# Sliding-window attention run inside the chunks of the first of two MLPs, with x kept on chip

## The reference

```python
# q, k, v: (4, 8, 576, 64) fp32; window 64
scores = q @ k.T / sqrt(64);  keep 0 <= i - j < 64, else -1e9
attn = exp(scores - max) / (sum + 1e-9);  o = attn @ v
x = o, heads beside each other: (2304, 512)
xn = x / sqrt(mean(x * x) + 1e-6) * rms_g
g = xn @ w_gate;  x2 = (g * sigmoid(g) * (xn @ w_val)) @ w_out     # 512 -> 1536 -> 512
h = x2 @ w_in;    out = (h * sigmoid(1.702 * h)) @ w_out2          # 512 -> 2048 -> 512
```

## Time and profile before

| | |
|---|---|
| runs | 1022.56, 1022.61, 1025.49 us |
| profiled execution, first to last instruction | 1025.4 us |
| PE busy | 982.7 us (96%) |
| DVE, ACT, POOL busy | 416.3, 349.5, 136.5 us |
| mean granted TensorE clock | 0.992 of 2.4 GHz |
| DMA | 58.29 MB, queue busy 20.2% of 16 engines' span |
| chain that ended last | PE 84%, DVE 7%, issue 4%, ACT 2%, DMA 1% |

### The profile page before, as it was taken

How to read it: one execution, slowest core, us unless ns; L and a number is a source line. 1 busy time by engine, 2 the same in 40 slices (tenths; PEclk the granted TensorE clock), 3 DMA queues, 4 the chain that set the end, 5 groups by cost and what they waited for, 6 DMA issues and landing times.

```text
span 1025.4 us, 15826 instructions
## 1 busy us (share of the span) xinstructions
PE 982.7 (96%) x5584; PEld 930.4 (91%) x5584; DVE 416.3 (41%) x797; ACT 349.5 (34%) x950; POOL 136.5 (13%) x90
## 2 busy tenths in 40 slices
PE   6887888999999999999999998999999999999998
PEld 5777778999999999999999997998999899999997
DVE  5989986653323332332333342222232322322322
ACT  5877876322112122122122342232232222322322
POOL 3343364620000000000001652000000000000000
PEclk9999999999999999999999998999999999999999
DMA  8656762512002002002003332010010010100000
GB/s 169 142 146 163 166 178 83 157 31 70 0 0 69 0 0 69 0 0 69 0 0 123 123 124 82 1 54 8 0 61 0 0 61 0 61 0 0 31 0 31
DMA packets 98603, 58.29 MB, mean 57 GB/s; under 512 B 59664, under 2 KB 90128, under 8 KB 98576
## 3 DMA queue, kind: packets, MB, share of 16 engines
q1 hardware_dynamic: 98576, 57.95, 20.2%
HBM read 42.60 MB, written 15.34 MB: 57 GB/s over the span
## 4 chain that ended last, share of the span: by engine, by line
PE 84%; DVE 7%; issue 4%; ACT 2%; DMA 1%; SPq 1%; DVEq 0%; POOL 0%; ACTq 0%
PE ps L589 21%; PE ps L591 21%; PE ps L590 21%; PE ps L674 6%; PE ps L676 6%; PE ps L675 6%; DVE nmax L882 1%; DVE probT L906 1%; DVE rrec L891 1%; DVE vwin L918 1%; ACT prob L718 1%; DVE prob L897 1%; DVE xT L244 1%; DVE rrec L894 1%; DMA wstage<-in_moe_w_out 1%
## 5 line engine op out<-in xcount | busy, mean ns | idle before, releaser
L589 PE MATMUL ps<-x_hi,w_main 128*128 128x384 f32 x672 | 226.2, 337 | 0.0
L591 PE MATMUL ps<-x_lo,w_main 128*128 128x384 f32 x672 | 225.6, 336 | 0.0
L590 PE MATMUL ps<-x_hi,w_main 128*128 128x384 f32 x672 | 225.5, 336 | 0.0
L1004 DVE TENSOR_TENSOR hid<-ps,sig 128x384 f32<-128x384 f32 x96 | 53.5, 558 | 295.1 <-ACT sig L835 295.0
L835 ACT ACTIVATE sig<-ps 128x384 f32<-128x384 f32 x96 | 47.2, 492 | 281.2 <-PE ps L591 281.2
L771 ACT ACTIVATE sig<-ps 128x384 f32<-128x384 f32 x72 | 35.4, 492 | 301.0 <-PE ps L591 301.0
L589 PEld LDWEIGHTS ps<-x_hi,w_main 128*128 128x128 f32 x672 | 126.5, 188 | 3.1
L590 PEld LDWEIGHTS ps<-x_hi,w_main 128*128 128x128 f32 x672 | 126.4, 188 | 2.8
L591 PEld LDWEIGHTS ps<-x_lo,w_main 128*128 128x128 f32 x672 | 126.4, 188 | 0.0
L970 DVE TENSOR_TENSOR sig<-ps,sig 128x384 f32<-128x384 f32 x72 | 40.1, 557 | 210.9 <-ACT sig L771 210.9
L589 PE MATMUL ps<-x_hi,w_tail 128*128 128x384 f32 x288 | 97.0, 337 | 0.0
(11 more groups left out here) (87 smaller groups left out, 1612.9 us busy)
## 6 DMA issues: line engine op xcount, KB each, us to landing
wstage<-in_moe_w_out SPq DMA_DIRECT2D x28, 256.0 KB, 3.5
xstage<-xs_scratch SPq DMA_DIRECT2D x6, 960.0 KB, 5.9
xs_scratch<-xT SPq DMA_DIRECT2D x16, 288.0 KB, 2.2
xs_scratch<-ostage SPq DMA_DIRECT2D x6, 768.0 KB, 3.9
xstage<-xs_scratch SPq DMA_DIRECT2D x6, 768.0 KB, 4.5
out_dram<-ostage SPq DMA_DIRECT2D x18, 256.0 KB, 2.0
qraw<-in_q SPq DMA_DIRECT2D x30, 144.0 KB, 3.0
kraw<-in_k SPq DMA_DIRECT2D x30, 144.0 KB, 3.2
```

What stands on the lines that cost most here:

```text
L589: pe.matmul(out_, w[:, 0, cols], xh, start=first, stop=False)
L590: pe.matmul(out_, w[:, 1, cols], xh, start=False, stop=False)
L591: return pe.matmul(out_, w[:, 0, cols], xl, start=False, stop=last)
L1004: nc.vector.tensor_tensor(hid[:, f % 2, :], ps[:, H_BANK + f % 2, 0:T], sig[:, f % 2, :], ALU.mult).then_inc(hidB_made, 1)
```

## The change

**Layout.** q, k, v and the weights are laid out on the host: q block-diagonal for its pair of heads (`q_bd`), k transposed (`k_t`), v as windows of 128 keys for each block (`v_win`), weights by chunk (`w_a`, `w_b`). The transposes of q and k on PE, their evictions on ACT and the copies of v on DVE are gone. The scale of 1/8 goes into the exponential and, by one more small DVE operation, into the row maximum.

**Attention.** A step has 256 queries (4 blocks of 64) of a pair of heads, across batch borders; there are 36. Only the first 4 steps (256 tokens) run before the MLPs. There POOL normalises. The other 32 run inside the chunks of the first four tiles of A, 8 a tile, in chunks 1 to 8: scores between gate and val, transposes before the projection, product with v after it. ACT loads the table of exponentials and that of the sigmoid once in each such chunk. In chunk 10 the sum of squares, the inverse norm and the scaling of the next tile follow.

**x.** Attention's output stays in `xT` in SBUF, is scaled in place, and isn't stored or loaded again. The x2 of A still goes through DRAM.

**Tiles.** A has tiles of 256, 512, 512, 512, 512 tokens, B 512, 512, 512, 512, 256. `sig` and `hid` are single, gate and val have one bank each, and `h_hi` and `h_lo` have three slots.

**Weights.** All twelve slots are split by POOL (cast, `weights_hi_A`, `weights_hi_B`) and DVE (subtraction, `weights_lo_A`, `weights_lo_B`), one of the three parts at a time, none on ACT.

All Python loops are unrolled, the evictions of x2 and of the output are shared by ACT and DVE, and `dynamic_dma_scratch_size` is 1024. The core of the diff, by parts:

```diff
-    GB = 3
...
-    T = 384
-    TILES = TOK // T
...
+GB = 4
...
+    TILES_A = ((0, 256), (256, 512), (768, 512), (1280, 512), (1792, 512))
+    TILES_B = ((0, 512), (512, 512), (1024, 512), (1536, 512), (2048, 256))
+    NA, NB = len(TILES_A), len(TILES_B)
+    TMAX = 512
+    EARLY = 4
...
+    SUMSQ_AT = 10
+    def steps_of(t):
+        return (0, EARLY) if t == 0 else (EARLY + 8 * (t - 1), EARLY + 8 * t)
...
+        w_all = sb("w_all", [P, CA * SLOT], F32R)
+        wstage = sb("wstage", [P, 2 * 3 * DM], F32)
+        x_hi = sb("x_hi", [P, DC, TMAX], F32R)
+        x_lo = sb("x_lo", [P, DC, TMAX], F32R)
...
+        xT = sb("xT", [P, DC, TMAX], F32)
+        h_hi = sb("h_hi", [P, RING, TMAX], F32R)
+        h_lo = sb("h_lo", [P, RING, TMAX], F32R)
+        sig = sb("sig", [P, TMAX], F32)
+        hid = sb("hid", [P, TMAX], F32)
...
+        def x2stage(t):
+            home = wstage if t < NA - 1 else late
+            return home[:, 0:DC * TMAX].rearrange("p (c t) -> p c t", c=DC)
...
+        def o_half(h, s):
             rows = slice(h * BLK, (h + 1) * BLK)
+            group, c = divmod(s, PAIRS)
+            t = 0 if group == 0 else (group + 1) // 2
+            at_ = group * GT - TILES_A[t][0]
+            src = ps[rows, o_bank(s), :].rearrange("p (n k) -> p n k", n=GB)[:, :, h * BLK:(h + 1) * BLK]
+            return t, c, at_, xT[rows, c, at_:at_ + GT].rearrange("p (n r) -> p n r", n=GB), src
+        def evacuate_o(eng, copy, h, s):
+            t, c, at_, dst, src = o_half(h, s)
+            eng.wait_ge(pv_done, s + 1)
+            wait(eng, x_hi_ready, DC * t)
+            wait(eng, x_lo_ready, DC * t)
...
+            def load_wA(c, m):
+                if c >= 2:
+                    sp.wait_ge(w_split, splitsA(c - 2, m))
+                sp.dma_start(raw(c % 2, m), w_a[c, :, m * DM:(m + 1) * DM]).then_inc(w_loaded[c % 2][m], 16)
...
+            for t in range(NA - 1):
+                first, last = steps_of(t + 1)
+                for c in range(CA):
+                    if t == 0 and c + 3 < CA:
+                        for m in range(3):
+                            load_wA(c + 3, m)
+                    s = first + c - FIRST_STEP
+                    if first <= s < last and s + 2 < STEPS:
+                        load_qk(s + 2)
+                    s -= 1
+                    if first <= s < last and s + 2 < STEPS:
+                        load_v(s + 2)
                 store_x2(t)
...
+            def normalise(s):
+                pool.wait_ge(rec_order, 2 * s + 2)
+                by = rrec[:, s % 2, :].rearrange("p (n o) -> p n o", o=1).to_broadcast([P, GB, P])
+                nc.gpsimd.tensor_tensor(prob[:, s % 2, :, :], prob[:, s % 2, :, :], by,
+                                        ALU.mult).then_inc(probs_normed, 1)
...
+            def weights_hi_A(c):
+                for m in range(3):
+                    pool.wait_ge(w_loaded[c % 2][m], 16 * (c // 2 + 1))
+                    nc.gpsimd.tensor_copy(slotA(c)[:, m, 0, :], raw(c % 2, m)).then_inc(w_hi_made, 1)
+            def weights_hi_B(f):
+                pool.wait_ge(projA_done, (NA - 1) * CA + last_slot_under(f) + 1)
+                for m in range(2):
+                    pool.wait_ge(w_loaded[f % 2][m], loadsB(f, m))
+                    nc.gpsimd.tensor_copy(chunkB(f)[:, m, 0, :], raw(f % 2, m)).then_inc(w_hi_made, 1)
...
+            normalise(0)
+            weights_hi_A(0)
+            for s in range(1, EARLY):
+                normalise(s)
+                squares(s - 1)
+            squares(EARLY - 1)
+            weights_hi_A(1)
+            weights_hi_A(2)
+            for t in range(NA - 1):
+                first, last = steps_of(t + 1)
+                for c in range(CA):
+                    s = first + c - FIRST_STEP - 2
+                    if first <= s < last:
+                        squares(s)
+                    if t == 0 and c + 3 < CA:
+                        weights_hi_A(c + 3)
...
+            scores(0)
+            for s in range(EARLY):
+                if s + 1 < EARLY:
+                    scores(s + 1)
+                transpose_probs(s)
+                probs_by_v(s)
+            sum_squares(0)
+            for t in range(NA):
+                first, last = steps_of(t + 1) if t + 1 < NA else (0, 0)
+                for c in range(CA + LAG):
                     if c < CA:
+                        gate(t, c)
+                        s = first + c - FIRST_STEP
+                        if first <= s < last:
+                            scores(s)
+                        val(t, c)
+                    s = first + c - FIRST_STEP - 1
+                    if first <= s < last:
+                        transpose_probs(s)
+                    if c == SUMSQ_AT and last:
+                        sum_squares(t + 1)
+                    if c >= LAG:
...
+                for c in range(CA):
+                    s = first + c - FIRST_STEP
+                    now = first <= s < last
+                    sigmoid_A(t, c)
+                    if now:
+                        nc.scalar.preload_act_table_set(EXP_SET)
+                        exponentials(s)
+                    hid_hi_A(t, c)
+                    if c == SUMSQ_AT and last:
+                        nc.scalar.preload_act_table_set(EXP_SET)
+                        inverse_rms(t + 1)
+                    if now or (c == SUMSQ_AT and last):
...
+            row_max(0)
+            for s in range(EARLY):
+                if s + 1 < EARLY:
+                    row_max(s + 1)
+                reciprocal_of_sum(s)
+                if s >= 1:
+                    evacuate_o(dve, nc.vector.tensor_copy, 0, s - 1)
+                evacuate_probT(s)
+            evacuate_o(dve, nc.vector.tensor_copy, 0, EARLY - 1)
+            weights_lo_A(0)
+            scale_x(0)
             dve.wait_ge(g_loaded, 16)
...
+            for t in range(NA):
+                first, last = steps_of(t + 1) if t + 1 < NA else (0, 0)
+                for c in range(CA):
+                    s = first + c - FIRST_STEP
+                    silu_A(t, c)
+                    if first <= s < last:
+                        row_max(s)
+                    hidden_A(t, c)
+                    if first <= s - 1 < last:
+                        evacuate_probT(s - 1)
+                    if first <= s < last:
+                        normalise(s)
+                    hid_lo_A(t, c)
+                    if first <= s - 1 < last:
+                        evacuate_o(dve, nc.vector.tensor_copy, 0, s - 1)
+                    if t == 0 and c + 2 < CA:
+                        weights_lo_A(c + 2)
+                    if c == SUMSQ_AT and last:
                         scale_x(t + 1)
+                    if t == NA - 1:
+                        for f in range(CB):
+                            if last_slot_under(f) == c - LAG - 1:
+                                weights_lo_B(f)
                 dve.wait_ge(val_done, CA * (t + 1))
...
```

More of the change, by code:

```diff
@@ L230, in evacuate_o, with splitsA @@
[L230 to L245 removed]
+        def splitsA(c, m):
+            return 3 * c + m + 1
@@ new lines, in _ @@
+            load_qk(0)
+            load_wA(0, 0)
+            load_v(0)
+            load_qk(1)
+            load_wA(0, 1)
+            load_v(1)
+            sp.dma_start(gcol[:, :], rms_g).then_inc(g_loaded, 16)
+            for s in range(2, EARLY):
+                load_qk(s)
+                load_v(s)
+                load_wA(0, 2) if s == 2 else load_wA(1, 0)
+            load_wA(1, 1)
+            load_wA(1, 2)
+            load_qk(EARLY)
+            load_v(EARLY)
+            load_qk(EARLY + 1)
@@ L423, in _ @@
[L423 to L428 removed]
+                then(nc.gpsimd.affine_select(out=mask[rows, 3, :], in_=mask[rows, 3, :],
+                                             compare_op=ALU.is_ge, fill=NEG, base=-BLK,
+                                             pattern=[[1, P]], channel_multiplier=0))
@@ L524, in scores, with transpose_probs @@
                                     start=False, stop=True, skip_group_check=True)
                 ins.then_inc(scores_done, 1)
-            def transpose_probs(b, kk):
-                there, j, n = behind(b, kk)
-                if not there:
-                    return
-                pe.wait_ge(probs_normed, n + 1)
-                wait(pe, probT_ready, n)
+            def transpose_probs(s):
+                pe.wait_ge(probs_normed, s + 1)
+                if s < EARLY:
+                    wait(pe, probT_ready, s - 1)
+                else:
+                    for h in range(2):
+                        pe.wait_ge(o_evacuated[h], s)
```

1103 lines of the change are left out of this document (440 added, 663 removed).

## The result

The kernel after takes 981.21 us (median of 4 runs, 979.64 to 981.89) beside 1024.05 for the kernel before on the same chip: ratio 0.9577, 95% interval 0.956 to 0.9594, 4.2% faster. The forecast was 1005 us with a range of 984 to 1026; the direction was right, the size was not, and the time lies 3 us under the range. The profiled execution has a span of 980.1 us.

The account below looks back on a forecast made before the run. PE bounds both MLPs, behind a serial attention of 155 us. Lead 40, MLP matmuls 851.3, steps 83.2, squares 4.0, first tile 20 and 2, tail 3.5, unexplained 4: 1008.0, scaled 1005 us; range 984 to 1026.

Parts of the forecast that it names:

- per column, wider is no cheaper: MLP matmuls: 0.450 and 0.453 ns a column at 384 and 512 columns, so re-tiling gains nothing; 851.3 us in all.
- The 256-column estimate by columns (0.115): MLP matmuls of the 256-token tiles: 0.115 us each, scaled by columns from 384; 624 of them.
- the addition of 1.9 us a chunk for the lock: First tile: POOL's squares and casts meet DVE's subtractions and exclude one another, making a chunk 8.9 us.
- my 20: First tile: PE stalls 17 us over eight chunks, plus 3 while the first splits fill; 20 us.
- the lower bound of 3: First tile's stall if POOL and DVE operations never meet: 3 us.
- about 5.3 each: Lead: the steps after the first, tied through PE's order, add 5.3 us each, from 17 to 33 us.
- The 4 us unexplained: Whole kernel: 1025.4 us profiled before against a calibration of 1021.1; the missing 4 us carried into the forecast.
- rival C: MLP stream: PE waits for normalised probabilities 1.0 us in each of 32 steps, giving 1037 us; chance 0.10.
- rival B: MLP matmuls: 256 columns run at the pace of 384, giving 1024 us; chance 0.08.
- Sums, tail: Sums of squares in the stream: 4.0 us; eviction and store at the end: 3.5 us instead of 3.8.
- the hole's going: Start of the second MLP: ACT's wait for weights goes, and the cold clock with it: 0 us instead of 7.
- rival A: First tile and lead: POOL and DVE interleave without harm, no stall, lead 36 us, scaled 984 us; chance 0.16.

Follow-up runs that it names:

- Fillers: Kernel after with matmuls whose result nobody reads added in the lead to keep PE busy: 974.06 us, ratio 0.9508.
- the new order: Kernel after with the lead's scores two steps ahead, DVE's reciprocal before the next row maximum, an earlier weight load, no filler matmuls: 969.88 us, ratio 0.9458.

## Why the prediction was wrong

**Fixed cost (13.7 of the 27.9 us: 16.8 too much for 512 columns, 3.1 too little for 256).** The step that failed is "per column, wider is no cheaper", worked out from nine matmuls at one place. The same trace held the other reading: in `w_tail` the same form ran at 227 ns, and 384 columns at 173 with 227 gives a constant of 11 to 13 ns. I took a disturbed pace for the pace of the form. A shift of 32 bytes makes the same disturbance in the kernel after; in the kernel before, the distance of `w_tail` brought `w_main` only to 231, so its cause is shown in part. The 256-column estimate by columns (0.115) was off the other way, by 5 ns. The narrow tiles in the second MLP show the constant directly.

The Trainium skill, page "TensorE: Matmul & The Clock Gate", section "Back-to-back issue gap", has the form N/2.4 GHz plus a constant, which I argued away. It gives 2.5 ns, for the isolated gap. The three paces here have this form with 13.3 ns, in a stream with a weight load for every matmul.

**First tile (14.3 us).** The step that failed is the addition of 1.9 us a chunk for the lock, on top of DVE's 7. DVE's work itself was about right: it is busy 12.27 of the 13.6 us from 66.6 to 80.2. But the lock fell more on POOL, which had slack. DVE lost 7.5 us in the whole tile instead of 15 in eight chunks, and from 66.6 to 80.2 its 6.1 us a chunk fit under PE's 6.8. The excess of 7.7 us is 2.2 of slow clock in the first chunk, waits of 1.38, 0.65 and 0.48 us up to 66 us, 2.3 in small ones after it (0.72 of them before the sum of squares), and 0.7 that I can't place. So the stall is some 5.5 us beside my 20; the lower bound of 3 was nearer. Moving a subtraction to POOL made this tile 2.3 us longer: the effect that I had feared, far smaller.

The Trainium skill, page "SBUF — State Buffer", section "Who interferes with whom", has the exclusive lock and says that the order of issue decides who waits. The trace agrees: POOL's operation began 0.15 us after DVE's first subtraction and took 2.20 us instead of 0.61. It waited for all three, though, not for one. It does not follow from the lock that DVE is the one that waits.

**Lead (6.2 us the other way).** The step that failed is "about 5.3 each", summed at full clock: I had doubled only the first scores for a cold PE. The first step ended at 16.9 us as forecast (17). The granted clock was 0.50 from 15 to 25 us, and the next three took 6.9 us each in the mean, 4.7 more in all; the work behind them took 8.5 us instead of 7. Fillers gave back 4.0 us of the lead and the new order 11.5: the term that I had as fixed was the largest thing still to be gained.

**The 4 us unexplained** of the calibration did not come back; the account of after closes within 0.5 us. The trace of before shows where they were: by the starts of its tiles, one of the first MLP takes 75.05 us where 432 x 0.173 gives 74.74, and one of the second 67.02 where 192 x 0.173 + 144 x 0.232 gives 66.62. Six of each make 4.3 us. So the residue was mainly the 384-column form running a little over 173 ns, a form that the change removes. To carry it forward added 4 us with no reason.

**Right.** A step costs 2.56 us against 2.6, all of it on the path: rival C (waits in the stream) did not come, with PE full from 127 us on. 256 columns do not run at the pace of 384 (rival B). Sums, tail and the hole's going were as forecast, but I had put the hole down to ACT's wait for weights alone; in the kernel after, casts on ACT make none, and in the kernel before some 1.4 us of it read as the lock. That stores and reloads of x were worth nothing follows from the account, which leaves no room for them; no run tried it by itself. Of rival A the small stall came true, its lead of 36 did not; the time near its 984 was made up by the pace.

**The range.** Its low end was one rival, not the sum of independent errors: pace, stall and residue could all fall the same way, and did. The low end with the 227 ns of `w_tail` for all 3360 matmuls would have been 17 us lower.

## What to carry to other kernels

Take the pace of a form from every place where it runs, fit width against time, and treat the remainder as a fixed cost of each matmul: wider tiles save it. Where two engines share a lock, ask which of them has slack and which issues without a gap before adding its price to the path. In a short serial stage in front of a full one, look first at the order of each engine's list: one step more of lookahead, with no operation of the next step ahead of one that is ready, takes waits and low clock together (here 11.3 us).

## What the runs showed of the hardware

- A stream of fp32r matmuls with a weight load each runs, where nothing disturbs it, at n/2.4 GHz + 13.3 ns: 120, 173 and 227 ns at 256, 384 and 512 columns.
- Shifting the h operand by 32 bytes took 512-column matmuls from 227 to 233 ns (6.7 us of the kernel). In some placements the first six or nine matmuls after a change of width take 224 to 236 ns and then settle at 227; in others (`w_tail` before) they run at 227 from the second on. The rule behind both is open.
- When DVE issues three operations back to back, a POOL operation started beside the first ends after the last (2.20 us instead of 0.61). Beside longer POOL work DVE is held too (two subtractions in 2.44 us instead of 1.27).
- With its waits in the lead shortened, PE was granted the upper level (2.4 GHz) from 10 to 30 us, where in the kernel after it had 0.66, and from 15 to 25 us 0.50, the lower one.
